# Where gates, high parts, weight splits and evictions stand in the short slots of a linear-attention and two-layer MLP kernel

## The reference, cut to what matters

```python
mag = np.sqrt(a_re * a_re + a_im * a_im)
scale = np.minimum(mag, 0.999) / (mag + 1e-06)
a_re_n, a_im_n = (a_re * scale, a_im * scale)
for t in range(S):                      # S = 768, batch 4, heads 8, D = 48
    new_re = ar * S_re - ai * S_im
    new_im = ar * S_im + ai * S_re
    S_re, S_im = (new_re + k v, new_im)
    y[:, :, t] = q S_re
h = x @ w_in;  g = h * clip(h + 3, 0, 6) / 6;  x = g @ w_out       # d_model 384, d_ff 2048
h = x @ w_in;  g = max(h, 0) + alpha * min(h, 0);  out = g @ w_out
```

## Time and profile before

| | us |
|---|---|
| median of 3 runs | 1003.45 |
| the profiled execution's own time | 1005.47 |
| its span | 1003.8 |
| TensorE (PE) busy | 961.2 (96%) |
| VectorE (DVE) busy | 583.0 (58%) |
| ScalarE (ACT) busy | 502.1 (50%) |
| GpSimd (POOL) busy | 269.9 (27%) |
| share of TensorE in the chain that ended last | 85% |

### The profile page before, as it was taken

How to read it: one execution, slowest core, us unless ns; L and a number is a source line. 1 busy time by engine, 2 the same in 40 slices (tenths; PEclk the granted TensorE clock), 3 DMA queues, 4 the chain that set the end, 5 groups by cost and what they waited for, 6 DMA issues and landing times.

```text
span 1003.8 us, 17714 instructions
## 1 busy us (share of the span) xinstructions
PE 961.2 (96%) x6786; PEld 864.6 (86%) x6786; DVE 583.0 (58%) x1049; ACT 502.1 (50%) x907; POOL 269.9 (27%) x251
## 2 busy tenths in 40 slices
PE   0899988999999999999999999999999999999998
PEld 0788988899999999999999998888888888888786
DVE  6767886867777767777662345444434444344332
ACT  7766877667877777776643443322222222222211
POOL 0000222222333322322222333332333333323232
PEclk9999999999999999999999999999999999999999
DMA  7753333332333332333320801023060060230000
GB/s 206 202 131 80 96 75 97 93 101 73 88 96 101 97 98 72 95 88 81 82 70 2 306 1 56 1 72 87 0 153 6 1 157 1 72 86 1 32 1 32
DMA packets 83589, 79.97 MB, mean 80 GB/s; under 512 B 32688, under 2 KB 78256, under 8 KB 83120
## 3 DMA queue, kind: packets, MB, share of 16 engines
q1 hardware_dynamic: 78384, 74.07, 27.7%
q10 hardware_dynamic: 5120, 4.76, 1.9%
HBM read 50.34 MB, written 9.44 MB: 60 GB/s over the span
## 4 chain that ended last, share of the span: by engine, by line
PE 85%; DVE 5%; ACT 3%; issue 2%; SPq 2%; DMA 1%; ACTq 0%; DVEq 0%
PE op L1262 12%; PE hp L1263 12%; PE op L1263 12%; PE hp L1262 12%; PE op L1264 12%; PE hp L1264 12%; PE yp L1250 3%; PE gp L1257 2%; PE hp L1285 2%; PE gp L1229 2%; PE yp L1229 2%; PE op L1310 2%; SPq L437 1%; PE tp L1238 1%; DMA st<-prod 1%
## 5 line engine op out<-in xcount | busy, mean ns | idle before, releaser
L572 POOL TENSOR_TENSOR g_lo<-gated,g_hi 128x512 fp32r<-128x512 f32 (+2 forms) x240 | 267.7, 1116 | 726.0 <-ACT g_hi L673 726.0
L673 ACT ACTIVATE g_hi<-gated 128x512 fp32r<-128x512 f32 (+2 forms) x240 | 126.3, 526 | 320.7 <-DVE gated L968 273.7
L964 DVE TENSOR_SCALAR gate<-hp,alpha_sb 128x512 f32<-128x512 f32 x96 | 72.0, 750 | 209.4 <-PE hp L1264 209.4
L953 DVE SCALAR_TENSOR_TENSOR gated<-gate,hp 128x256 f32<-128x256 f32 (+1 forms) x160 | 75.2, 470 | 134.2 <-ACT gate L666 133.8
L1262 PE MATMUL op<-g_hi,wb_hi 128*128 128x256 f32 (+1 forms) x432 | 137.3, 318 | 3.3 <-ACT out_sb L678 2.0
L1262 PE MATMUL hp<-x_hi,wa_hi 128*128 128x256 f32 (+1 forms) x432 | 134.7, 312 | 1.8 <-DVE gated L953 1.5
L1264 PE MATMUL op<-g_hi,wb_lo 128*128 128x256 f32 (+1 forms) x432 | 132.5, 307 | 0.0
L1263 PE MATMUL op<-g_lo,wb_hi 128*128 128x256 f32 (+1 forms) x432 | 132.3, 306 | 0.0
L1264 PE MATMUL hp<-x_hi,wa_lo 128*128 128x256 f32 (+1 forms) x432 | 132.2, 306 | 0.0
L1263 PE MATMUL hp<-x_lo,wa_hi 128*128 128x256 f32 (+1 forms) x432 | 132.2, 306 | 0.0
L666 ACT ACTIVATE gate<-hp,half 128x256 f32<-128x256 f32 (+1 forms) x160 | 81.1, 507 | 93.1 <-PE hp L1264 80.9
(11 more groups left out here) (113 smaller groups left out, 1645.9 us busy)
## 6 DMA issues: line engine op xcount, KB each, us to landing
st<-prod SPq DMA_DIRECT2D x64, 145.1 KB, 3.1
raw<-a_in SPq DMA_DIRECT2D x4, 2304.0 KB, 15.1
a_sb<-a_in SPq DMA_DIRECT2D x24, 288.0 KB, 3.9
qk_sb<-qk_in SPq DMA_DIRECT2D x24, 288.0 KB, 3.5
st<-prod ACTq DMA_DIRECT2D x32, 145.1 KB, 2.6
v_pad<-v_in SPq DMA_DIRECT2D x24, 192.0 KB, 3.6
x_raw<-x SPq DMA_DIRECT2D x6, 768.0 KB, 16.2
out<-out_sb SPq DMA_DIRECT2D x5, 768.0 KB, 4.2
```

Of the source, the lines that this page charges most:

```text
L572: pool.tensor_tensor(g_lo[:, at, 0:wide], gated[:, at * UT:at * UT + wide], g_hi[:, at, 0:wide].bitcast(F32), ALU.subtract).then_inc(glo_d ...
L673: act.activation(g_hi[:, at, 0:wide], gated[:, at * UT:at * UT + wide], ACT.Copy).then_inc(ghi_done, 1)
L953: dve.scalar_tensor_tensor(out=gated[:, to], in0=gate[:, at], scalar=1.0, in1=hp[:, n % 2, 0:wide], op0=ALU.min, op1=ALU.mult).then_inc(ga ...
L964: dve.tensor_scalar(gate[:, at], hp[:, n % 2, 0:wide], 0.0, alpha_sb[:, m:m + 1], ALU.min, ALU.mult).then_inc(gate_done, 1)
```

## The change

In short slots the order within an item changes on two engines. On ScalarE, behind gate_of(n+2) and the copies of k, now come high(n+2), the splits and leave (behind_gate), and only then the chunk's own steps; at c the table load of logs stands in front of them. On VectorE gate1(n+2) stands in front of phases and fractions, and the two masks in front of backward. Long slots keep their order. Weight splits are planned by split_plan: one or two for each item, three for every two items, from item 1 to item 16, a block when the first unit has read it (usable); they are now also called in the three items alone.

```diff
@@ -76,9 +76,27 @@
 
 A_BLOCKS = [[(0, k, q) for k in range(KT_DM)] for q in range(NQ)]
 B_BLOCKS = [(1, n) for n in range(NWI)]
-W_ORDER = [b for q in range(NQ) for b in A_BLOCKS[q] + B_BLOCKS[(0, 1, 3, 6)[q]:(1, 3, 6, NWI)[q]]]
-
-W_ITEM = 3
+
+
+
+
+def usable(block):
+
+    return -(-(block[1] + 1) * WPC // DM) if block[0] else block[2] * WPC // P + 1
+
+
+def split_plan():
+    left = [b for q in range(NQ) for b in A_BLOCKS[q]] + B_BLOCKS
+    plan = {}
+    for n in range(1, 2 * MT_FF):
+        plan[n] = [b for b in left if usable(b) <= n][:1 + n % 2]
+        left = [b for b in left if b not in plan[n]]
+    assert not left
+    return plan
+
+
+SPLIT_PLAN = split_plan()
+W_ORDER = [b for n in SPLIT_PLAN for b in SPLIT_PLAN[n]]
 NRP = 12
 RP = WSZ // NRP
 RAW_ITEMS = range(4, 10)
@@ -139,7 +157,7 @@
 
 def splits_at(n):
 
-    return range(max(0, n - W_ITEM), min(max(0, n + 1 - W_ITEM), len(W_ORDER)))
+    return [W_ORDER.index(b) for b in SPLIT_PLAN.get(n, [])]
 
 
 def split_count(blocks):
@@ -591,8 +609,8 @@
                 act.wait_ge(a_landed[c % 2], 48 * (c // 2 + 1))
                 act.activation(t_sq[:, :, :, :], a_sb[:, c % 2, :, :, :], ACT.Square).then_inc(squares_set, 1)
 
-            def logs(c):
-                if c > 0:
+            def logs(c, loaded=False):
+                if c > 0 and not loaded:
                     act.preload_act_table_set("natural_log_exp_and_others")
                 act.wait_ge(m2_done, c + 1)
                 need(act, inv_done, c)
@@ -734,24 +752,39 @@
             gate_of(0)
             gate_of(1)
             squares(4)
+            def behind_gate(n):
+                if n + GSTEP >= MT_FF:
+                    high(n + GSTEP)
+                for w in splits_at(n):
+                    split_w(w)
+                if n % MT_FF == MT_FF - 1:
+                    leave(n // MT_FF)
+
             for n in range(ALONE):
                 gate_of(n + GSTEP)
+                for w in splits_at(n):
+                    split_w(w)
                 if n == 0:
                     angle(3)
 
             for steps, n, c0, c1, c2, c3 in places():
                 keeps = not is_last(c0)
                 gate_of(n + GSTEP)
-                if "a" in steps:
-                    if keeps:
-                        copy_k(c0, 0)
-                    if c1 is not None:
-                        waves(c1)
-                if "c" in steps:
-                    if keeps:
-                        copy_k(c0, 1)
-                    if c2 is not None:
-                        logs(c2)
+                if "a" in steps and keeps:
+                    copy_k(c0, 0)
+                if "c" in steps and keeps:
+                    copy_k(c0, 1)
+
+                if is_short(c0):
+                    if "c" in steps and c2 is not None:
+                        act.preload_act_table_set("natural_log_exp_and_others")
+                    behind_gate(n)
+                    if "c" in steps and c1 is not None:
+                        copy_ends(c1)
+                if "a" in steps and c1 is not None:
+                    waves(c1)
+                if "c" in steps and c2 is not None:
+                    logs(c2, is_short(c0))
                 if "s" in steps and c3 is not None:
                     squares(c3)
                 if "v" in steps and c2 is not None:
@@ -762,14 +795,13 @@
                         stack(c1)
                 if "k" in steps and c2 is not None:
                     angle(c2)
-                if n + GSTEP >= MT_FF:
-                    high(n + GSTEP)
-                if "c" in steps and c1 is not None:
-                    copy_ends(c1)
-                for w in splits_at(n):
-                    split_w(w)
-                if n % MT_FF == MT_FF - 1:
-                    leave(n // MT_FF)
+                if not is_short(c0):
+                    if n + GSTEP >= MT_FF:
+                        high(n + GSTEP)
+                    if "c" in steps and c1 is not None:
+                        copy_ends(c1)
+                    if n % MT_FF == MT_FF - 1:
+                        leave(n // MT_FF)
             for n in range(N1 - MT_FF, NT):
                 u, m = divmod(n, MT_FF)
                 if n + GSTEP < N1:
@@ -1046,21 +1078,29 @@
             gate1(2)
             for n in range(1, ALONE):
                 gate1(n + GSTEP)
+                for w in splits_at(n):
+                    split_w(w)
 
             for steps, n, c0, c1, c2, c3 in places():
+                if is_short(c0):
+                    gate1(n + GSTEP)
                 if "a" in steps and c1 is not None:
                     phases(c1)
                     fractions(c1)
                     if "B" in steps:
                         forward(c1)
-                gate1(n + GSTEP)
+                if not is_short(c0):
+                    gate1(n + GSTEP)
+                elif "f" in steps:
+                    mask(c0, 0)
+                    mask(c0, 1)
                 if "c" in steps and c1 is not None:
                     backward(c1)
                 if "d" in steps and c1 is not None:
                     with_qk(c1)
                 if "e" in steps and c1 is not None:
                     product(c1, 0)
-                if "f" in steps:
+                if "f" in steps and not is_short(c0):
                     mask(c0, 0)
                     mask(c0, 1)
                 if "g" in steps and c1 is not None:
```

## The result

The changed kernel takes 1031.11 us (median of 4 runs, 1029.04 to 1034.36) against 1004.78 for the kernel before, measured beside it: a ratio of 1.0269, 95% interval 1.0249 to 1.0289. It is slower, as forecast, but by 26 us and not by 15, and beyond the upper end of the range, 1026.

The account below looks back on a forecast made before the run. TensorE bounds the kernel, with the ScalarE-VectorE loop just below; the change makes that loop 23.1 us. Short slots +12.9 and first long slot 2 make +14.9 us on the median 1003.45: 1018, range 1001 to 1026.

Parts of the forecast that it names:

- The bound: TensorE bounds the kernel at 21.04 us per slot; without splits the ScalarE-VectorE loop is only 0.7 us per slot short.
- the loop: Chunk steps passed between ScalarE and VectorE, fractions to next fractions: 20.3 us without splits, 23.1 after the change, at most 24.0.
- Gates and high parts: Short slots: early high parts wait for gate1, holding up the chunk's steps behind them; a seven-item slot takes 23.1 us.
- the walk: Links of the ScalarE-VectorE loop added in the new order, fractions to fractions, in slot 9 times: 23.1 us against TensorE's 21.04.
- the last link: gate_of of item a to gate1 0.50, to the phases 0.33, phases and fractions 2.2: 3.0 us.
- the span's sum: Short slots 257.1 us instead of 244.2, so +12.9; 2 more at the first long slot; total +14.9 us.
- The splits: Ten more in the first unit, 6 us on VectorE; slot 4 up to 2 us late, taken as 0; 4.2 us leave slot 4's loop.
- rival C: GpSimd collisions at their bound, or a first unit short of VectorE time: 8 to 10 us more, 1027; 0.05 with D.
- A: Rival: loop stays hidden at 21.04 us, slots 4 to 8 gain, -10 to -13 us, 992; chance 0.13.
- B: Rival: loop near 21.9 us, slots 4 to 8 gain some 7, the six after lose some 6: 1003; chance 0.12.
- D: Rival: more TensorE waits bring the lower clock, about 1.7 us each time, adding nothing unless C holds; 0.05 with C.
- The signs: Slots 9 to 13 at 22.5 to 24 us; ScalarE's gated waits up 20 us or more; TensorE waiting mostly for stacked products.

Follow-up runs that it names:

- the control: Kernel before, with GpSimd's low part cut to 16 of 256 columns in the short slots: 998.30 us, ratio 0.9937.

## Why the prediction was right or wrong

- **The bound.** Right: the change made the loop the bound. The 0.7 us per slot that it lacked by my count was rather some 0.3, an estimate with the phases at 1.67 us and not at 1.23; gate1 alone in front, with slots at 21.2 us, fits that.
- **Gates and high parts.** Right in place and nearly in size. The links of the walk against the trace (ends and starts as the prediction has them): fractions to the gate of d 5.2 and 5.2; gate of d to the inverses 3.9 and 3.9; both gate1 links and the table load as said. The sum is 23.1 against 23.6. What is missing lies in one link: the phases with their fractions take 2.66 us (232.74 to 235.40) where I put 2.2, because a low part runs beside them.
- **The step that failed** is the size of the collisions of VectorE's steps with a low part, which I put at nothing. Outside the walk it is the sentence "between 0 and 0.3 us for each of some three more steps of a slot, at most 1 us per slot; I take 0". Inside the walk it is the last link, "phases and fractions 84.59 to 86.81, 2.2". All other links were read in slot 9, but this one in slot 3, in the first unit, where GpSimd has no low part and the three scans take 1.23 us. Slot 9 of the kernel before had them at 1.67 already:

```profile
243.31 1.67 DVE L845 TENSOR_TENSOR_SCAN t_phase<-ones,t_frac,t_dt 128x128 f32<-128x128 f32 x3
```

They take 1.67 us in the changed kernel too, so the loop is 23.6 us and not 23.1. Of the 9.8 us that the span's sum lacked, slots 4 to 14 have 7.5, and a loop 0.5 us longer makes 5.5 of them in eleven slots. The steps that collide only in the new order also cost more than the 0 to 0.3 us that I had allowed: the backward scan takes 1.66 us instead of 1.23, the forward scan 1.55 instead of 1.05, the squares' sum 1.09 instead of 0.55. But in slots 9 and 10 VectorE idles 0.66, 0.77 and 1.09 us behind them for a gate, so there they lengthen no link of the loop. I let the sum stand on 0 although a rule spoke against it: by the sentence on the Trainium skill ("SBUF — State Buffer", section "Who interferes with whom") the sum was 8 us higher, at 1026. The trace agrees with that rule, 1.67 against 1.23 us for three scans with a low part beside them and without one. The 8 was itself short: 0.3 us for three steps in eleven slots is up to 10.
- **The splits.** "I take 0 and keep the 2 for the range" failed too, on the small side: slot 3 took 1.9 us more. ScalarE's timeline of the changed kernel at that place:

```profile
100.90 0.62 ACT L701 ACTIVATE wa_hi<-wa_raw 128x512 fp32r<-128x512 f32 x1
...
101.42 0.62 ACT L701 ACTIVATE wa_hi<-wa_raw 128x512 fp32r<-128x512 f32 x1
...
101.94 0.48 ACT L673 ACTIVATE x_hi<-yp 128x384 fp32r<-128x384 f32 x1
```

Two splits stand in front of x_high, and the first hidden product of the second unit waits 1.9 us for x_lo. With the splits behind x_high that wait was 0.5 us in the run with the plan alone and 1.3 us in the one with the masks, and slot 3 took 25.2 us in both, 1.3 longer than before. So most of the delay comes from the plan and not from this place; by which way is not shown. In the later slots the splits did give back what was said, 6.4 us by the profiles when tried alone.
- **The range.** The loop's upper bound of 24.0 us in eleven slots would have given 1028 and not 1026, and rival C, collisions with a late first unit, said 1027 with a chance of 0.05. What came is the forecast's mechanism and C together. They are not rivals: a longer loop is what lets collisions count, as the control shows. I should have added them instead of setting one against the other.
- **A, B and D.** A and B are out. D played no part that the traces show. The changed kernel's mean clock was 0.993 against 0.997, but most of this is a stretch from 38 to 46 us, ahead of all that the change touches (first the changed kernel, then the one before):

```profile
38.00:42.00 4.00, 2.97 (x14) 2.98 (x15) 1.82 (x5) 0.79 (x3) 0.00 (x0) 0.50 0.87 240
```

```profile
38.00:42.00 4.00, 4.00 (x20) 4.00 (x21) 2.58 (x6) 1.05 (x5) 0.00 (x0) 1.00 0.94 270
```

It cost nothing: from there to slot 2 it is 22.66 us (39.03 to 61.69), and 22.65 before. In the short slots each kernel has one stretch at the lower clock, at about 168 and 200 us.
- **The signs.** Slots 9 to 13 at 23.8 us and ScalarE's waits for gated (26.3 us before, 62.9 after, 60 to 560 us) came as said. TensorE's waits did not: I had said mostly for stacked products, with some for gated, and it is 3.8 us against 16.2. The wait for an eviction is not gone either, 1.3 us where 2.0 were.
- **What remains open.** Slot 14 took 26.3 us, 1.9 more than its eight items give by my loop. VectorE's fractions there are 24.2 us apart (353.48 to 377.65), as the loop says, but I had priced the eighth item by the loop alone (1.3 us), and TensorE's own work for eight items was 24.1 us in the kernel before, to which 1.7 us of waits come here, 1.4 of them for gated. That these waits come on top is my reading. The effect of the wait, apart from that of the place, was not isolated.

## What to carry to other kernels

An engine's order that looks urgent-first can be wrong when the urgent step waits for an answer to what was issued just before it: leave something between question and answer. Walk the loop between the engines once in the new order, from start to start, and compare it with the period of the engine that bounds the kernel; if they are within a few per cent, every added wait and every slowed instruction counts in full, and unknown costs should be added at their rows' size, not at zero. Read every link in the same stretch: a row from a stretch where another engine rests can lack a collision.

## What the runs showed of the hardware

A wait of TensorE need not be long for its clock to fall. Stretches of the changed kernel and of the one with the high part an item later (busy time by engine, granted clock, DMA share), each behind waits of 1.90 and 1.01 us, and of 2.22 us:

```profile
165.00:167.00 2.00, 1.34 (x9) 1.14 (x9) 2.00 (x6) 1.99 (x3) 0.21 (x1) 1.00 0.00 0
167.00:170.00 3.00, 2.54 (x17) 2.30 (x21) 1.63 (x4) 2.48 (x7) 0.53 (x1) 0.57 0.39 131
205.00:207.00 2.00, 1.62 (x15) 1.62 (x16) 1.93 (x5) 1.97 (x3) 0.92 (x1) 1.00 0.73 197
```

```profile
263.00:266.00 3.00, 3.00 (x14) 3.00 (x15) 2.19 (x4) 1.83 (x4) 1.53 (x1) 0.50 0.00 0
```

0.50 is the 1.2 GHz level. The wait of 1.51 us that ends at 205.38 left the clock at 1.00, while one of 1.57 us in the kernel before was followed by 0.50; so a wait's length alone doesn't tell. In the kernel with the high part an item later even waits of 2.44 and 2.66 us, ending at 144.31 and 287.58 us, were followed by 1.00.
